# Up-projections of two MLPs as seven products of half blocks, with the weights in the outer loop

## What is computed

```python
# attention, per batch (2) and head (8), 768 tokens, 64 columns
mask = q_assign[:, :, :, None] == k_assign[:, :, None, :]     # nearest of 16 centroids
attn = softmax(where(mask, q @ k.T / 8, -1e9));  out = attn @ v
x = out.transpose(0, 2, 1, 3).reshape(1536, 512)
# MLP 1: w_in 512 x 2048, w_out 2048 x 512
h = x @ w_in
g = np.where(h >= 1, h, np.where(h <= -1, 0.0, (h + 1) ** 2 / 4))
x = g @ w_out
# MLP 2: w_gate, w_val 512 x 1536, w_out 1536 x 512
xn = x / sqrt(mean(x * x) + 1e-6) * rms_g
y = (silu(xn @ w_gate) * (xn @ w_val)) @ w_out
```

## Time and profile before

| | us |
|---|---|
| median of 3 runs (lowest, highest) | 855.99 (855.37, 860.15) |
| the profiled execution, its own time | 861.13 |
| its span in the trace | 859.1 |
| PE busy | 824.1 (96%) |
| DVE busy | 523.0 (61%) |
| ACT busy | 355.6 (41%) |
| POOL busy | 214.7 (25%) |

### The profile page before, as it was taken

One profiled execution on the slowest core, in us unless ns is written; L12 is line 12 of the kernel. 1 busy time (PEld: TensorE's weight loads), 2 busy tenths in 40 slices (PEclk: granted clock), 3 DMA queues, 4 the chain that ended last, 5 costly groups with the idle time before them and its releaser, 6 DMA issues.

```text
span 859.1 us, 12427 instructions
## 1 busy us (share of the span) xinstructions
PE 824.1 (96%) x4231; PEld 697.5 (81%) x4231; DVE 523.0 (61%) x863; ACT 355.6 (41%) x618; POOL 214.7 (25%) x150
## 2 busy tenths in 40 slices
PE   4899999999999899999999999999999999999997
PEld 4798898898887688888888888788888888888886
DVE  4798898898897577344334586674445434363333
ACT  3788878887877412232223212331114211141111
POOL 0123333333376499000000276680000000000000
PEclk9999999999999999999999999999999999999999
DMA  6779556546430260000000223330001000010001
GB/s 138 162 203 193 115 120 144 122 108 144 112 83 10 76 212 1 1 0 0 0 0 0 72 76 98 91 105 1 0 1 49 0 0 0 0 49 0 0 0 50
DMA packets 64960, 54.44 MB, mean 63 GB/s; under 512 B 29600, under 2 KB 52128, under 8 KB 64928
## 3 DMA queue, kind: packets, MB, share of 16 engines
q1 hardware_dynamic: 64928, 54.05, 25.2%
HBM read 27.30 MB, written 3.15 MB: 35 GB/s over the span
## 4 chain that ended last, share of the span: by engine, by line
PE 64%; DVE 2%; ACT 1%; issue 0%; ACTq 0%; DVEq 0%
PE ps L626 23%; PE ps L604 15%; PE ps L593 14%; PE ps L637 11%; DVE vb L974 1%; DVE gl L982 1%; ACT tb L753 0%; DVE gb L978 0%; PE ps L498 0%; PE ps L469 0%; DVE xsl L939 0%; DVE xr L1032 0%; PE ps L611 0%; PE ps L612 0%; ACT xsh L736 0%
## 5 line engine op out<-in xcount | busy, mean ns | idle before, releaser
L626 PE MATMUL ps<-xsh,w2h 128*128 128x512 f32 x288 | 112.0, 389 | 0.0
L626 PE MATMUL ps<-xsl,w2h 128*128 128x512 f32 x288 | 112.0, 389 | 0.0
L626 PE MATMUL ps<-xsh,w2l 128*128 128x512 f32 x288 | 112.0, 389 | 0.0
L753 ACT ACTIVATE tb<-ps,half 128x512 f32<-128x512 f32 x48 | 33.1, 690 | 184.9 <-PE ps L593 184.9
L844 DVE TENSOR_SCALAR_CACHE_REDUCE sf<-ps 128x768 f32<-128x768 f32 x96 | 91.2, 951 | 28.2 <-PE ps L458 27.5
L674 ACT ACTIVATE pbuf<-sf,minn 128x768 f32<-128x768 f32 x96 | 89.8, 935 | 22.1 <-DVE sf L844 22.1
L853 DVE TENSOR_TENSOR ptl<-ps,pth 128x512 fp32r<-128x512 f32 x144 | 95.5, 682 | 5.0 <-ACT pth L664 4.8
L664 ACT ACTIVATE pth<-ps 128x512 fp32r<-128x512 f32 x144 | 84.5, 589 | 31.6 <-PE ps L482 19.9
L781 ACT ACTIVATE tb<-tb 128x512 f32<-128x512 f32 x36 | 22.8, 633 | 165.2 <-DVE tb L1007 165.2
L1007 DVE TENSOR_TENSOR tb<-ps,ub 128x512 f32<-128x512 f32 x36 | 24.9, 691 | 108.4 <-PE ps L626 108.3
L482 PE MATMUL ps<-ident,pbuf 128*128 128x128 f32 x576 | 85.1, 273 | 1.4 <-ACT pbuf L674 1.0
(11 more groups left out here) (111 smaller groups left out, 1656.3 us busy)
## 6 DMA issues: line engine op xcount, KB each, us to landing
q<-atile SPq DMA_DIRECT2D x32, 192.0 KB, 3.7
k<-atile SPq DMA_DIRECT2D x32, 192.0 KB, 3.6
w1raw<-in_moe_w_in SPq DMA_DIRECT2D x16, 256.0 KB, 5.1
w1raw<-in_moe_w_out SPq DMA_DIRECT2D x16, 256.0 KB, 6.2
nat<-in_q SPq DMA_DIRECT2D x16, 192.0 KB, 3.7
nat<-in_k SPq DMA_DIRECT2D x16, 192.0 KB, 3.9
q<-btile SPq DMA_DIRECT2D x16, 192.0 KB, 3.2
k<-btile SPq DMA_DIRECT2D x16, 192.0 KB, 4.0
```

Of the source, the lines that this page charges most:

```text
L626: last = pe.matmul(bank(f % 2 * 2 + b), w[:, f, o:o + P], x[:, kt, :], start=(kt == 0 and i == 0), stop=(kt == KT - 1 and i == 2))
L753: act.activation(tb[:, f % 2, :], bank(f % 4), ACT.Relu, bias=half[:, :], scale=0.5)\
```

## The change

Up-projections are done by a seven-product scheme (Strassen's, in Winograd's form). The weight block, the chunk of x and the result are each cut in 2 x 2: K in halves of 256 (KH = 2 tiles of 128), the tokens of a chunk in halves of 256 (HC), and the hidden columns in two blocks of 128. In MLP 1 these are blocks 2q and 2q + 1; in MLP 2 block q of w_val and block q of w_gate. Eight products of half blocks become seven, of sums and differences of the operands.

- POOL makes the seven left operands of each weight from its four parts, by four sums (`sum_up`), and splits them (`high_up`, `low_up`): 1792 elements a partition. For each chunk and MLP the seven operands of x are made and split too: four sums on POOL (`t_sum`), the high part on ACT (`t_hi`), the low part on DVE (`t_lo`); for the very first, chunk 0 of MLP 1, POOL makes the low part (`first_t_lo`) and ACT the high part, within attention's last blocks.
- A step is one q and one chunk; there are 60 (24 and 36). The order is: a pair of q outermost, then the 3 chunks, then the two q of the pair. Up weights have three slots, down weights two (MLP 1) or four. The results of a pair are added to xr by DVE (`take_y`), after every second step.
- Four of the products are left in PSUM, or read and then added onto: ACT copies the first three out (`snap`), then products 5 to 7 are accumulated onto the same banks, and DVE adds the parts up (`combine`).
- Down products are as many as before, and one step behind the up products.
- The norm's factor is applied to the gate (`scale_gate`) and, transposed by PE, to the output of MLP 2. Sums of squares are prepared by ACT (`squares`) and POOL (`prepare`).
- All loops of the dense part are unrolled, and SBUF is laid out anew.

```diff
+            def up(s):                                   # PE
...
+                if c == 0:
+                    pe.wait_ge(up_split, q + 1)
...
+                for j, (dst, opened) in enumerate(((BANK_A, True), (BANK_C, True), (BANK_D, True), (BANK_B, True),
+                                                   (BANK_A, False), (BANK_C, False), (BANK_D, False))):
...
+                    if s and j in (1, 2):
+                        pe.wait_ge(combined, 5 * (s - 1) + 3 + j)
+                    if not opened:
+                        pe.wait_ge(snapped, 3 * s + j - 3)
+                    for kt in range(KH):
+                        for i, (a, b) in enumerate(((wh, th), (wh, tl), (wl, th))):
+                            last = pe.matmul(dst[:, 0:HC], a[w][:, j, kt, :], b[c][:, j, kt, :],
...
+            for s in range(NS + 1):
+                if s < NS:
+                    up(s)
+                if s in NORM_AT:
+                    sum_squares(NORM_AT.index(s), s)
+                if s in TURN_AT:
+                    turn_inverse(TURN_AT.index(s), s)
+                if s:
+                    down(s - 1)
...
+            for s in range(NS):                          # ACT
+                mlp = STEPS[s][0]
+                snap(s, 0)
+                snap(s, 1)
...
+                snap(s, 2)
...
+                copy_corner(s)
...
+                else:
+                    silu(s)
...
+                    hidden_hi(s, 0)
+                if s == 2:
+                    t_hi(2)
+                if s in SUMS_AT:
+                    sums_hi(SUMS_AT.index(s))
+                if s in SPLIT_AT:
+                    t_hi(3 + SPLIT_AT.index(s))
+                if s in SQUARES_AT:
+                    squares(SQUARES_AT.index(s))
...
+                else:                                    # DVE, a step of MLP 2
+                    combine(s)
+                    scale_gate(s)
+                    take_y(s - 1, 0)
+                    product(s)
+                    take_y(s - 1, 1)
+                    hidden_lo(s, 0)
+                    take_y(s - 1, 2)
+                    take_y(s - 1, 3)
...
+            def load_up(q):                              # SP
+                s = q % 3
+                if q >= 3:
+                    sp.wait_ge(up_products, PROD * (LAST[q - 3] + 1))
...
+        SQUARES_AT = (20, 22, 24)
+        SUMS_AT = (21, 24, 26)
+        NORM_AT = (22, 25, 27)
+        INVERSE_AT = (23, 25, 27)
+        SPLIT_AT = (22, 24, 26)
+        TURN_AT = (26, 28, 30)
```

More of the change, by code:

```diff
@@ L100, in build @@
+        curve = [place(f"curve{i}", [P, 2, CH], F32, G0, (4 * i + 2) * CH * 4) for i in range(2)]
         ident = place("ident", [P, P], F32, C0)
@@ L156, in build @@
+        eqr = place("eqr", [P, 2 * NT, NC], F32, O10, 2 * HB + 768)
+        mskin = place("mskin", [P, NT, 2 * NC], F32R, C0, 1664)
+        zt = [place(f"zt{c}", [P, TPC], F32, C0, 2432 + 32 * c) for c in range(3)]
         ps = [ctx.enter_context(nc.psum_tensor(f"ps{i}", [P, 2, 512], F32)) for i in range(4)]
```

898 lines of the change are left out of this document (544 added, 354 removed).

## The result

The changed kernel takes 930.53 us (median of 4 runs, 928.83 to 933.5) where the kernel before takes 857.59 on the same chip (855.37 to 860.15): a ratio of 1.085, 95% interval 1.081 to 1.090. It is slower, as forecast, but by 73 us where the forecast was 41, and 5.5 us above the range. The profiled execution has a span of 930.0 us.

A forecast was written before the change was run, and what follows sets the result against it. TensorE, busy 96% of 859.1 us, was taken as the bound. 819.5 without stalls + 24 start + 5 first MLP + 22 between MLPs + 28 second MLP + 1.7 end = 900.2 span; + 2.0 - 5.1 = 897 us, range 842 to 925.

The forecast's parts named there:

- no-stall sum: Whole span without any stall: dense part starts at 287.5, matmuls take 527.4, last copy and store 4.6; 819.5 us.
- (d): Rival: up-projections are bound by weight loads, 0.188 us each, so the span is past 990 before any stall; chance 0.02.
- (b): Rival inside the main case: up matmuls cost the lower bound, 0.1134 us; 12 us less, 885; chance 0.15.
- The mutual exclusion: Dense part: GpSimd operations and VectorE operations with both inputs in SBUF exclude each other, alternating one instruction each.
- the mark of an error: Whole run: the prediction calls itself wrong if TensorE's snap waits are under 10 us in all.
- The start: First dense steps: TensorE waits for the second up weight, then for VectorE's low parts and hidden_low; 24 us (8 to 32).
- ten bursts of 2.8: Second MLP: ten GpSimd weight preparations delay VectorE's product and stall TensorE about 2.8 us each; 28 us (10 to 48).
- the forecast's chain: Second-MLP step: VectorE's late product delays ScalarE's copy, next step's snap stands behind it, product 5 waits; 1.5 us spare.
- Between the MLPs: Steps 20 to 30: operations inserted in ScalarE's and VectorE's queues delay snaps; 19 us, 22 with half-clock stretches (8 to 35).
- second count: Second-MLP step: VectorE needs 5.7 us of 7.7 and loses 2.4 to GpSimd; 8.1, more than TensorE needs.
- (a): Rival: bursts fall into VectorE's idle time, all stalls stay below 39.6 us; faster, 830 to 845 us; chance 0.20.
- (c): Rival: each stall over 1.85 us brings a half-clock stretch, 17 us, with upper bounds; 925 to 945 us; chance 0.10.

The follow-up runs named there:

- e2_pieces: The changed kernel with each up weight's low part made in seven subtractions of 256 elements in place of one of 1792; ratio 1.041 to the kernel before.
- e3_no_fill: The changed kernel with up weights from the fourth on neither loaded nor prepared, so the output is another; ratio 1.027 to the kernel before.
- e5: e2_pieces with squares, high and low parts of the second MLP's chunks one step later in ScalarE's and VectorE's queues; ratio 1.035 to the kernel before.
- e16: e2_pieces with a third queue order between the MLPs, gain on ScalarE, and work of VectorE, GpSimd and ScalarE there cut; ratio 1.009 to the kernel before.
- e4: The changed kernel with useless matmuls into free columns filling nine of TensorE's waits; ratio 1.080 to the kernel before.

## Why the prediction was right in sign and short in size

**The direction, and the no-stall sum.** It forecast 819.5 without stalls. Measured: 287.2 + 2520 x 0.120 + 228.5 + 1.5 + 3.3 = 822.9. The price of a matmul was 0.120, not 0.118: 5.0 us more, 1.3 less at the end. Weight loads didn't bind (d), and the price of (b), 0.1134, is not it.

**The mutual exclusion.** GpSimd's wl was forecast at 4.3 us and takes 4.24; operations of VectorE with two SBUF inputs have means of 0.66 to 1.34 and reach 4.5, those that read PSUM kept theirs. Snap waits are 54.2 us, far over the 10 named as the mark of an error. What follows from holds as long as a whole operation is shown by e2_pieces: 37 us less of span for 46 us more of GpSimd. By the Trainium skill, "SBUF — State Buffer", SBUF: two separate sides, the shared port pair is locked for the whole instruction. The trace agrees: 4.50 us for a low part of 0.68 beside a GpSimd operation of 4.33.

**The start**: 24 forecast, 26.0 measured. The first wait came as drawn (5.9 us before step 1, forecast 6.5). The rest is right in size only: it was to be waits for the low parts of chunk 1 and for hidden_low, and it was 2.4 us for those low parts and then 9.6 and 2.6 for snaps in steps 2 and 3, behind VectorE.

**The MLPs.** GpSimd's low parts start in steps 5, 8, 11, 14 and 17, then 20, 23, 27, 29 and 30, then in seven steps from 35 to 53. So the ten bursts of 2.8 that make the prediction's 28 are those of steps 27 to 53, and three of them fall between the MLPs. For steps 31 to 59 it forecast 7 x 2.8 = 19.6, and 21.9 were measured besides the end (1.7 forecast, 1.2 measured). For steps 6 to 19 it forecast 4.2 (5 less the burst of step 20), and 4.9 were measured. e3_no_fill shows that the bursts make both losses (2.2 and 0.3 stay), and the timeline of step 36 above shows the forecast's chain. This step of the prediction holds, mechanism and price.

**Between the MLPs**: this is the step that failed. "Sum 19, with half-clock stretches 22", and for the bursts in that stretch 0.8 + 3 x 2.8 = 9.2 more, makes 31.2; measured were 53.2 (54.7 less the norm's matmuls). These 22.0 us are most of the miss of the span, 29.8: the no-stall sum adds 3.4, the start 2.0, the two MLPs 3.0, and the end takes 0.5 off. The prediction counted what ScalarE's inserted operations put off, snap by snap, as if VectorE kept up, and took a burst there for as cheap as in a quiet step.

The runs split the 53.2. The five bursts cost 22.7 (e3), 4.5 each, where 9.2 were forecast; pieces recover 13.7 of them. Everything else costs 30.5, where 22 were forecast. The snap waits that the prediction counted exist (25.2 us), but e5 took them away (1.8 stay) and gained 3.8: the time came back at the next wait. TensorE's idle time there is 34.8 us in 11 waits. VectorE is busy for 133.5 us there beside 99.0 us of matmuls, holds included, and still for 106.8 in e3, without the bursts: three times low parts and reciprocals on top of the steps' own work. The second count in the prediction (busy time of VectorE against that of TensorE) was made for a step of the second MLP and not for this stretch; there it came out too high, 8.1 us a step where 198.0 / 29 = 6.8 were measured, and here it would have warned.

In the order of the experiments: pieces take 13.7 us of the 54.7, another order about 5, then VectorE's added work 10, or with GpSimd's and ScalarE's 18.8, and 17.0 stay in e16, of which 1.5 is the norm. TensorE's waits in e16 are

```profile
PE ps L695 <- ACT z L929: 2.0, 1, 2.0
PE ps L739 <- DVE snap L1103: 2.0, 3, 0.9
PE ps L695 <- issue: 2.0, 1, 2.0
PE ps L695 <- ACT snap L872: 1.6, 2, 1.2
PE ps L695 <- ACT zt L934: 1.2, 1, 1.2
```

8.8 us together, and 6.8 us ran at half clock. Why these waits stay was not settled: a chain of waits through the short steps 24 to 28 may need more than 7.8 us a step by itself; e16 doesn't exclude it.

**Rivals.** (a) needed stalls under 39.6 us; they were 107, and still 60 in e3, with none of the 17 later bursts. (c) gave 925 to 945 and the time fell there, but not by its mechanism: the time at half clock did rise, to 41.3 us in steps 20 to 30 alone, but with 28.7 us less of it e4's span is only 3.6 us shorter. Nor did each stall over 1.85 us bring such a stretch: waits of 2.11, 2.18 and 2.11 us before 731, 828 and 838 brought none, waits of 2.74 and 1.98 before 773 and 785 did. That 930.5 lies in (c)'s range is luck.

The last 3.6 us of the miss lie in the conversion to the median: 3.1 were taken off for the profiled execution of before, and after it was 0.5 more than its span.
